# Attention outputs written channels by time in two 64-column halves of the PE array, their last rows placed by small DMAs

## What is computed

```python
# q, k, v, alpha: (4 batches, 8 heads, 768 steps, 48 channels)
for t in range(S):
    state = alpha[:, :, t, :, None] * state + einsum('bhd,bhe->bhde', k[:, :, t], v[:, :, t])
    y[:, :, t] = einsum('bhd,bhde->bhe', q[:, :, t], state)
x = y.transpose(0, 2, 1, 3).reshape(3072, 384)
x = (((x @ w1) * (x @ w2)) @ w3) @ w_out              # 384 -> 1024 -> 1024 -> 384
for e in range(4):                                    # p: the tokens' shares of the experts
    out += p[:, e:e + 1] * (np.maximum(x @ w1[e], 0) @ w2[e])
```

## Time and profile before

| | |
|---|---|
| median of 3 runs | 1300.9 us (1299.86, 1300.90, 1301.36) |
| span of the profiled execution | 1299.8 us |
| PE busy | 1274.5 us (98%), 6954 matmul instructions |
| PEld / DVE / ACT / POOL busy | 1170.7 / 525.1 / 310.5 / 290.5 us |
| granted TensorE clock, mean | 0.996 of full speed |
| attention outputs (L880, L884), PE busy in the records | 32.8 and 54.0 us |
| transposes of the outputs (L891) | 72 instructions, 12.3 us |

### The profile page before, as it was taken

How to read it: one execution, slowest core, us unless ns; L and a number is a source line. 1 busy time by engine, 2 the same in 40 slices (tenths; PEclk the granted TensorE clock), 3 DMA queues, 4 the chain that set the end, 5 groups by cost and what they waited for, 6 DMA issues and landing times.

```text
span 1299.8 us, 18234 instructions
## 1 busy us (share of the span) xinstructions
PE 1274.5 (98%) x6954; PEld 1170.7 (90%) x6954; DVE 525.1 (40%) x1160; ACT 310.5 (24%) x581; POOL 290.5 (22%) x236
## 2 busy tenths in 40 slices
PE   7989999999999998999999999999999999999999
PEld 4679999999999997999999999999999999999998
DVE  6786868777797311222222222222222222222222
ACT  2343333433343421111111111111111111111111
POOL 4455435444354623000000000000000000000000
PEclk9999999999999999999999999999999999999999
DMA  7432222323224231111111111111111111221101
GB/s 243 100 80 51 75 73 49 85 49 76 70 49 102 74 141 55 65 65 65 65 65 65 65 65 65 65 65 65 66 65 65 65 65 49 74 73 70 61 16 49
DMA packets 45725, 93.12 MB, mean 72 GB/s; under 512 B 3808, under 2 KB 14560, under 8 KB 45664
## 3 DMA queue, kind: packets, MB, share of 16 engines
q1 hardware_dynamic: 45664, 92.34, 23.8%
HBM read 78.17 MB, written 14.16 MB: 71 GB/s over the span
## 4 chain that ended last, share of the span: by engine, by line
PE 87%; DVE 7%; issue 2%; ACT 2%; POOL 1%; DMA 1%; DVEq 0%; SPq 0%; POOLq 0%
PE bank L845 27%; PE bank L844 27%; PE bank L846 27%; PE bank L884 2%; DVE inputs L618 1%; DVE decay L631 1%; DVE keys_t L642 1%; PE bank L880 1%; POOL inputs L390 1%; DMA inputs<-akq 1%; PE bank L865 1%; ACT h_hi L472 1%; DVE scores L648 1%; PE bank L891 1%; PE bank L949 1%
## 5 line engine op out<-in xcount | busy, mean ns | idle before, releaser
L810 DVE SCALAR_TENSOR_TENSOR h_lo<-bank,h_hi 128x512 fp32r<-128x512 f32 x192 | 132.7, 691 | 620.4 <-ACT h_hi L586 620.4
L586 ACT ACTIVATE h_hi<-bank 128x512 fp32r<-128x512 f32 x192 | 114.8, 598 | 667.9 <-PE bank L846 667.9
L845 PE MATMUL bank<-we_lo,h_hi 128*128 128x384 f32 x768 | 257.1, 335 | 0.0
L846 PE MATMUL bank<-we_hi,h_lo 128*128 128x384 f32 x768 | 256.9, 335 | 0.0
L844 PE MATMUL bank<-we_hi,h_hi 128*128 128x384 f32 x768 | 256.3, 334 | 0.0
L844 PE MATMUL bank<-x_hi,we_hi 128*128 128x512 f32 x576 | 227.0, 394 | 3.2 <-issue 3.2
L845 PE MATMUL bank<-x_lo,we_hi 128*128 128x512 f32 x576 | 228.8, 397 | 0.0
L846 PE MATMUL bank<-x_hi,we_lo 128*128 128x512 f32 x576 | 228.1, 396 | 0.0
L384 POOL TENSOR_TENSOR we_lo<-staged,we_hi 128x512 f32 (+1 forms) x48 | 61.4, 1305 | 533.2 <-ACT we_hi L457 533.0
L844 PEld LDWEIGHTS bank<-we_hi,h_hi 128*128 128x128 f32 x768 | 144.3, 188 | 9.1
L845 PEld LDWEIGHTS bank<-we_lo,h_hi 128*128 128x128 f32 x768 | 144.2, 188 | 8.2
(11 more groups left out here) (85 smaller groups left out, 1483.9 us busy)
## 6 DMA issues: line engine op xcount, KB each, us to landing
x_hi<-x_hi_spill SPq DMA_DIRECT2D x24, 768.0 KB, 4.9
x_lo<-x_lo_spill SPq DMA_DIRECT2D x24, 768.0 KB, 6.5
staged<-wset SPq DMA_DIRECT2D x60, 256.0 KB, 6.4
inputs<-akq SPq DMA_DIRECT2D x48, 288.0 KB, 4.5
values<-v_rows SPq DMA_DIRECT2D x24, 192.0 KB, 4.9
x_hi_spill<-x_hi_out SPq DMA_DIRECT2D x8, 576.0 KB, 3.4
x_lo_spill<-x_lo_out SPq DMA_DIRECT2D x8, 576.0 KB, 4.8
w_sb<-w_t SPq DMA_DIRECT2D x16, 256.0 KB, 9.2
```

The source lines that it names most:

```text
L586: act.activation(h_hi[:, s % 2, :], bank[s % 2][:, :], ACT.Relu).then_inc(h_hi_ready, 1)
L810: dve.scalar_tensor_tensor(out=h_lo[:, s % 2, :], in0=bank[s % 2][:, :], scalar=0.0, in1=h_hi[:, s % 2, :], op0=ALU.max, op1=ALU.subtract) ...
L845: pe.matmul(dst, left[0], right[1], start=False, stop=False)
L846: return pe.matmul(dst, left[1], right[0], start=False, stop=last)
```

## The change

The products of `outputs` swap their sides: the weights are now 64 columns of `decayed` or `values` and the moving side is 128 columns of queries or scores, so that the result comes out channels by time. The even head of a pair goes to partitions 0 to 63 of bank 7 and the odd head to 64 to 127. A head has 48 channels and a half 64 places: host code pads the values with zeros to 64 (the load of a chunk's values grows from 192 to 256 KB), and a pair's four groups of 128 columns fill the bank. `y_copy`, `turn_outputs` and `y_sb`'s place are gone. ACT and DVE write pairs 0 to 2 directly into `x0`, and pair 3 into a buffer `rest`, from which six DMAs a chunk (each 16 partitions, high and low part, 16 KB) carry it to the unused partitions 48 to 63 and 112 to 127 of the three pairs; the rows of w1 and w2 are permuted on the host to match. `up1` of a tile now waits for these DMAs (`x0_moved`). The branch for gates out of range, which does not run on this data, is adapted too. The diff, cut to its core:

```diff
+REST = ODD - D
+MOVED = 16 * 6
+VD = HEADS * ODD
 ...
-        values = sb("values", [P, 2, DM], F32, first)
+        values = sb("values", [P, 2, VD], F32, first)
         keys_t = sb("keys_t", [P, PAIRS, P], F32, first)
-        y_sb = sb("y_sb", [P, DM], F32, first)
         state = sb("state", [PD, PAIRS, 2 * D], F32, first)
-        decayed = sb("decayed", [PD, PAIRS, 2 * D], F32, first)
+        decayed = sb("decayed", [PD, PAIRS, 2 * ODD], F32, first)
 ...
+        rest = sb("rest", [P, 2, CHUNK], F32R, first)
+        rest_hi, rest_lo = rest[:, 0], rest[:, 1]
 ...
+        x0 = [sb(f"x0_{t}", [P, 2, KT, TILE1], F32R, first) for t in range(TILES1)]
+        x0_hi, x0_lo = [x[:, 0] for x in x0], [x[:, 1] for x in x0]
 ...
+            def move_rest(b, c):
+                sp.wait_ge(x0_lo_ready, CHUNKS * b + c + 1)
+                t, i = divmod(c, CHUNKS1)
+                at = slice(i * CHUNK, (i + 1) * CHUNK)
+                for k in range(KT):
+                    for row in range(2):
+                        sp.dma_start(x0[t][row * ODD + D:(row + 1) * ODD, :, k, at].bitcast(F32),
+                                     rest[row * ODD + k * REST:row * ODD + (k + 1) * REST, :, :].bitcast(F32)).then_inc(x0_moved, 16)
 ...
             load_chunk(0, 2)
+            move_rest(0, 0)
             load_pieces(0, 1)
 ...
                 load_chunk(into_b, into_c)
+                move_rest(b, c)
 ...
             load_after(BATCH - 1, 3, BATCH - 1, 5)
-            for q in range(PIECES // 2):
+            load_pieces(1, 0)
+            move_rest(BATCH - 1, 4)
+            load_pieces(1, 1)
+            load_pieces(1, 2)
+            move_rest(BATCH - 1, 5)
+            for q in range(3, PIECES // 2):
                 load_pieces(1, q)
 
-            sp.wait_ge(x0_lo_ready, BATCH * CHUNKS)
+            sp.wait_ge(x0_moved, MOVED * BATCH * CHUNKS)
 ...
-            def y_copy(b, c):
+            def x0_high(b, c):
                 act.wait_ge(y_done, CHUNKS * b + c + 1)
-                act.activation(y_sb[:, :], bank[7][:, 0:DM], ACT.Copy).then_inc(y_ready, 1)
-
-            def x0_high(b, c):
-                act.wait_ge(y_turned, CHUNKS * b + c + 1)
                 t, i = divmod(c, CHUNKS1)
-                act.activation(x0_hi[t][:, :, i * CHUNK:(i + 1) * CHUNK],
-                               bank[7][:, 0:DM].rearrange("p (k t) -> p k t", k=KT), ACT.Copy).then_inc(x0_hi_ready, 1)
+                y = bank[7][:, :].rearrange("p (a t) -> p a t", a=PAIRS)
+                act.activation(x0_hi[t][:, :, i * CHUNK:(i + 1) * CHUNK], y[:, 0:KT], ACT.Copy)
+                if not (isinstance(b, int) and b == 0 and c == 0):
+                    act.wait_ge(x0_moved, MOVED * (CHUNKS * b + c))
+                act.activation(rest_hi, y[:, KT], ACT.Copy).then_inc(x0_hi_ready, 1)
 ...
                     if chunk and s % 2:
-                        y_copy(*chunk)
                         x0_high(*chunk)
 ...
+                    dve.tensor_tensor(new_state, new, decayed[:, :, :].rearrange("p a (r e) -> p a r e", r=2)[:, :, :, 0:D],
+                                      ALU.add).then_inc(state_summed, 1)
 ...
-                    dve.tensor_tensor(decayed[rows, :, cols], state[rows, :, cols],
+                    dve.tensor_tensor(decayed[rows, :, row * ODD:row * ODD + D], state[rows, :, cols],
 ...
-                dve.tensor_tensor(x0_lo[t][:, :, at], bank[7][:, 0:DM].rearrange("p (k t) -> p k t", k=KT), x0_hi[t][:, :, at],
-                                  ALU.subtract).then_inc(x0_lo_ready, 1)
+                y = bank[7][:, :].rearrange("p (a t) -> p a t", a=PAIRS)
+                dve.tensor_tensor(x0_lo[t][:, :, at], y[:, 0:KT], x0_hi[t][:, :, at], ALU.subtract)
+                dve.tensor_tensor(rest_lo, y[:, KT], rest_hi, ALU.subtract).then_inc(x0_lo_ready, 1)
 ...
+                    heads = values[:, c % 2, pair * 2 * ODD:(pair + 1) * 2 * ODD].rearrange("p (r e) -> p r e", r=2)[:, :, 0:D]
+                    mm = pe.matmul(bank[7][0:PD, pair * 2 * D:(pair + 1) * 2 * D].rearrange("p (r e) -> p r e", r=2),
+                                   keys_t[:, pair, 0:PD], heads, start=True, stop=True)
 ...
+                    tiles = [bank[7][row * ODD:(row + 1) * ODD, pair * CHUNK:(pair + 1) * CHUNK] for row in range(2)]
                     if c >= 1:
-                        pe.matmul(bank[7][:, pair * 2 * D:(pair + 1) * 2 * D], inputs[:, c % 2, Q, pair, :], decayed[:, pair, :],
-                                  start=True, stop=False)
+                        for row in range(2):
+                            pe.matmul(tiles[row], decayed[:, pair, row * ODD:(row + 1) * ODD], inputs[:, c % 2, Q, pair, :],
+                                      start=True, stop=False)
                     for row in range(2):
-                        at = slice((2 * pair + row) * D, (2 * pair + row + 1) * D)
-                        mm = pe.matmul(bank[7][:, at], scores[:, pair // 2, pair % 2 * 2 + row, :], values[:, c % 2, at],
-                                       start=(c == 0), stop=(c == 0 or row == 1))
+                        at = slice((2 * pair + row) * ODD, (2 * pair + row + 1) * ODD)
+                        mm = pe.matmul(tiles[row], values[:, c % 2, at], scores[:, pair // 2, pair % 2 * 2 + row, :], start=(c == 0), stop=True)
                 mm.then_inc(y_done, 1)
-
-            def turn_outputs(b, c):
-                pe.wait_ge(y_ready, CHUNKS * b + c + 1)
-                for k in range(KT):
-                    mm = pe.transpose(bank[7][:, k * P:(k + 1) * P], y_sb[:, k * P:(k + 1) * P], identity[:, :])
-                mm.then_inc(y_turned, 1)
 
             def up1(b, s, which, wait_x0):
                 t, f = divmod(s % STEPS1, FT)
                 if which == 0:
                     if f == 0 and wait_x0:
-                        pe.wait_ge(x0_lo_ready, CHUNKS * b + CHUNKS1 * (s // FT + 1))
+                        pe.wait_ge(x0_moved, MOVED * (CHUNKS * b + CHUNKS1 * (s // FT + 1)))
 ...
-            steps = (score, state_products, outputs, turn_outputs)
-            first_beside = {4: (0, 1), 5: (2,), 6: (3,)}
-            second_beside = {3: (1, 0, 1), 6: (1, 2), 8: (1, 3), 18: (2, 0, 1), 22: (2, 2), 25: (2, 3)}
+            steps = (score, state_products, outputs)
+            first_beside = {4: (0, 1), 5: (2,)}
+            second_beside = {3: (1, 0, 1), 6: (1, 2), 18: (2, 0, 1), 22: (2, 2)}
 ...
+    v_rows = np.pad(v_rows, ((0, 0), (0, 0), (0, 0), (0, REST))).reshape(BATCH * CHUNKS, P, VD)
+    x0_rows = [(2 * k + row) * D + i if i < D else (2 * KT + row) * D + k * REST + i - D
+               for k in range(KT) for row in range(2) for i in range(ODD)]
 ...
-        "wset0": weight_set(moe_w1, moe_w2),
+        "wset0": weight_set(moe_w1[x0_rows], moe_w2[x0_rows]),
```

More of the change, by code:

```diff
@@ L40 @@
 KT, FT = DM // P, FF // P
+assert REST * KT == D and KT == PAIRS - 1
 ALPHA_LOW, ALPHA_HIGH = 0.75, 1.0
@@ L117, in gated_attention_experts @@
         wp_lo = sb("wp_lo", [P, FT, DM], F32R, first)
-        x0_hi = [sb(f"x0_hi{t}", [P, KT, TILE1], F32R, first) for t in range(TILES1)]
-        x0_lo = [sb(f"x0_lo{t}", [P, KT, TILE1], F32R, first) for t in range(TILES1)]
+        x0 = [sb(f"x0_{t}", [P, 2, KT, TILE1], F32R, first) for t in range(TILES1)]
+        x0_hi, x0_lo = [x[:, 0] for x in x0], [x[:, 1] for x in x0]
         a_sb = sb("a_sb", [P, 2, TILE1], F32, first)
@@ L149, in gated_attention_experts @@
         redo_product = scores[0:PD, :, :, :].rearrange("p i a t -> p (i a t)")[:, 0:SEQ]
+        y_sb = keys_t[:, :, :].rearrange("p a t -> p (a t)")[:, 0:DM]
         redo_y = values[:, :, :].rearrange("p i d -> p (i d)")[:, 0:CHUNKS * 2 * D].rearrange("p (c e) -> p c e", c=CHUNKS)
@@ L182, in gated_attention_experts @@
         y_done = sem("y_done")
-        y_ready = sem("y_ready")
-        y_turned = sem("y_turned")
         x0_hi_ready = sem("x0_hi_ready")
         x0_lo_ready = sem("x0_lo_ready")
+        x0_moved = sem("x0_moved")
         a_done = sem("a_done")
@@ L528, in _ @@
             split_high(0, 1)
-            y_copy(0, 0)
             x0_high(0, 0)
@@ L535, in _ @@
             check(0, 2)
-            y_copy(0, 1)
             fold_high(4)
@@ L543, in _ @@
             check(0, 3)
-            y_copy(0, 2)
             pieces_high(0, 4)
@@ L577, in _ @@
                             act.wait_ge(redo_turned, CHUNKS * b + c)
-                        act.dma_start(y_sb[:, :], redo_dram[:, c].rearrange("p a e -> p (a e)")).then_inc(redo_y_loaded, 16)
+                        y_rows = y_sb.rearrange("p (k r e) -> p k r e", k=KT, r=2)
+                        act.dma_start(y_rows[:, :, :, 0:D].rearrange("p k r e -> p (k r) e"),
+                                      redo_dram[:, c, 0:KT].rearrange("p a (r e) -> p (a r) e", r=2)).then_inc(redo_y_loaded, 16)
+                        for row in range(2):
```

(20 more changed lines are left out.)

8 lines of the change are left out of this document (5 added, 3 removed).

## The result

The changed kernel takes **1338.3 us** (median of 4 runs, 1337.4 to 1339.2) against 1301.1 (4 runs, 1299.9 to 1302.3): ratio 1.028, 95% interval 1.027 to 1.030. It is 37 us slower. The forecast was 8 us slower, 1309, with a range to 1325; the sign was right and the size was not.

The account below looks back on a forecast made before the run. PE, busy 98% of the span, was taken as the bound, with DVE second beside the attention. Second tiles +0.9, first tiles +3.4 and the start +3.8 summed to +8.1 us, giving 1309.0 us, range 1294 to 1325.

Parts of the forecast that it names:

- The transposes and the waits for `y_sb`: Work removed on PE: 7.9 us of transposes and 5.8 us of waits, 13.7 us at the most.
- The halves overlap: Output products on PE: both array halves work at once, block 1.94 us, saving 0.66 us a chunk.
- rival B: Output products' halves run one after the other: block 3.5 us, total 1318 us; chance 0.12.
- The second subtraction on DVE: In each `x0_low` on DVE, the added subtraction was taken to cost 0.2 us.
- the signs: What would show the forecast right, among them DVE without idle before `g_product` beside chunks 0 to 2.
- Rival A: Moves take no more than PE's own road, so no wait at tiles: -13 us, 1288; chance 0.17.
- The start: First tile: chunk 2's `x0_low` ends at 72.45, moved at 76.3 against 73.20; 3.1 + 3.5 clock - 2.8 waits, +3.8 us.
- The lag, 3.85 us: From `x0_lo` to `x0_moved`: five issues of 0.35 us on SP plus a 2.1 landing, ends 2.8 and 5.0.
- rival C: Clock falls at the seven later tile boundaries too, 3.5 us each: three falls 1319, all 1333; chance 0.15.
- The step that what is queued behind that wait waits "for later events anyway": SP's queue behind the wait for `x0_lo_ready`: tile stores or next chunk's loads wait for later events anyway; no cost counted.
- Second tiles: Boundary of each batch's second tile, four of them: 1.4 us sooner, lag +1.63, net +0.2 each, +0.9 in all.
- First tiles: First tile of the next batch, three of them: 0.25 us sooner, lag +1.38, net +1.1 each, +3.4 in all.

Follow-up runs that it names:

- e1_no_moves: Changed kernel without the six small DMAs a chunk, SP only passing the semaphore on, output incomplete: 1291.0 us, ratio 0.993 to the kernel before.
- e7_early_x0: Changed kernel with e3_piece_order's load order, and ACT and DVE writing `x0` and `rest` earlier in each chunk: 1293.5 us, ratio 0.9955 to the kernel before.
- e4_fill_wait: Changed kernel with unread matmuls on PE before each wait for `x0_moved`, 18 in the loop and 36 at the start: 1327.6 us.
- e3_piece_order: Changed kernel with SP issuing the last batch's weight-piece loads ahead of the moves of chunks 3, 4 and 5: 1325.1 us.
- e6_half_moves: Changed kernel with only the even heads' three of six moves per chunk, output incomplete: 1306.9 us, ratio 1.005 to the kernel before.
- e9_one_half_at_a_time: e7_early_x0 with all output products of one head of the pairs ahead of the other's, instead of alternating: 1312.4 us.

## Why the prediction went wrong

*Right.* The sign, and its mechanism: PE's savings are real and are spent on waiting for the moves. The transposes and the waits for `y_sb` went. The halves overlap: 1.77 us and the edges, 1.91 in all, where 1.94 was forecast, so rival B is out. The second subtraction on DVE costs 0.2 us (`rest` ends at 128.31, `x` at 127.55 + 0.56 = 128.11). DVE's two idle times beside chunks 0 to 2 (0.32 and 0.53 us) are gone, as the signs said. Rival A's working, without the lag, gave 1288; e1_no_moves measured 1291.0 and e7_early_x0 1293.5.

*The start, right by luck.* PE's first matmul of tile 1 came 3.6 us late, where 3.1 was forecast for it (3.8 with the clock and the waits that absorb part), and the first of its next `up1` 3.4 late (82.49 against 79.12). But `rest` ended at 71.26 and not at 72.45, and the lag there was 5.5 us and not 3.85: two errors that cancel. What the clock alone cost there, for which 3.5 was forecast, isn't shown: with the clock kept up (e4_fill_wait) tile 1 starts 1.8 us later and is 3.5 shorter.

*The lag, 3.85 us.* It was built as five issues of 0.35 and a landing of 2.1. The landing was near enough (1.8), the issue was not: 0.63. The measured lag is 5.2, above even the upper end of 5.0. The nearest row was a load of another kind, and that the issue "could be nearly free" was a guess in the wrong direction. At eight boundaries this is 8 x 1.35 = 11 us.

*The clock, rival C.* The forecast had the clock fall at the start alone, with rival C at 0.15. It fell at five of the six boundaries in the loop with a wait of 3.5 us, and in the last batch. The forecast's wait of 2.45 us lay between a row without a fall and a row with one; the real one, 3.5 us with the longer lag, no longer lay between. Rival C's price for one fall, 3.5 us, was too high for the loop: it was taken from a stretch of light work, and e4_fill_wait shows 1.6 to 1.9 each, 8.3 in all. C with its price at all seven would have given 1333 and came nearest, but partly by luck: the price was twice the real one and stood in for the lag and for SP's queue.

*SP's queue in the last batch.* The step that what is queued behind that wait waits "for later events anyway" holds in the loop and fails behind it, where the queue holds weight pieces that wait for nothing that is late. The prediction looked at `load_pieces` at the start and not at the end. It cost 13 us by e3_piece_order: lag, clock and pieces of that boundary, and the stretch behind it.

*The sum, mended.* Second tiles: forecast +0.2, and 1.35 for the lag and 1.6 for the clock make 3.2; measured 2.6 (with the clock's fall of the start in it), 3.6 and 4.1 for the first three. First tiles: 1.1 + 1.35 + 1.6 = 4.1; measured 4.1, 4.2, 4.2. Over the run: 8.1 as forecast, 10.8 for the lag, 8.3 for the clock, and 7.9 for the last batch (8.6 less the 0.2 and 1.35, and the 0.8 behind it) make 35.1 of the measured 35.8. So the working of PE's savings against DVE's pace stands within about 1 us a tile; two terms and one place were missing.

*And where the moves stood.* The prediction took the end of `x0_low` as given and asked how long the DMAs are. In the kernel before 2.2 to 2.5 us lay behind it, and nothing asked for more. The outputs stood in their bank at about 122 us, though, and `x0_low` ended at 128.3 behind 16 transposes of 5.3 us that, as e7_early_x0 shows, can wait. With the order changed on ACT and DVE the issues and landings cost nothing at the boundaries of the loop; the start keeps its wait of 6.4 us.

## What to carry to other kernels

A transfer that is put between two engines needs its lead time moved ahead with it: look not only at the slack before the consumer, but at how long the data have been ready before the producer got to them, and put the producer's step there. Count small DMAs one by one on the queue that issues them, at the price of their own kind, and read that queue's program to its end. A wait that lowers the clock costs more than it seems: here most waits of 3.5 us were followed by slow work that cost another 1.6 to 1.9, and waits of 1.5 us before the same tiles were not, so the first microseconds taken off such a wait are worth the most.

## What was not expected of the hardware

- Issuing a 16 KB transfer from SBUF to SBUF takes SP 0.63 us; a load of 192 KB takes 0.35, and one of 256 KB in the changed kernel as well. One run per partition instead of two changes it to 0.61, half the partitions to 0.73. It lands 1.8 us after its issue (median of 144; 2.7 in e7_early_x0). By the Trainium skill, "DMA: Bandwidth & Descriptors", on the anatomy of a DMA issued by GpSimd, a transfer has some 2.0 us fixed, most of it at the receipt of the write, and the sequencer's dispatch is about 0.05 of it. These are issued by SP: the landing is near the page's figure, the issue is twelve times its dispatch.
- Idle PE and the clock, in rows of this case: after waits of 1.5 us (e6_half_moves) and 1.0 us (e3_piece_order) the granted clock stayed at 1.00; after 3.51 us PE's records show the 1.2 GHz level from 133.49 to 136.85. The length of one wait doesn't decide it alone: after 3.45 us at 421.82, and after 3.50 us in e3_piece_order (307.39), the clock did not fall, and in e6_half_moves it fell after 2.48 us (442.23).
- Two halves of 64 columns run float32 products at once, with the same 128 or 112 rows in both. The Trainium skill, "TensorE: Matmul & The Clock Gate", part 3, ties the overlap of a weight load with a running matmul to different row groups; 32 loads and 32 streams in 1.77 us speak against that here.
- Where the order of the queue changes from one half to the other (e9_one_half_at_a_time, 122.70), four records of `decayed` start from 122.70 on, ahead of the four of `values` at 122.92: the first product of the second half starts beside the last `decayed` product of the first, although a `values` product stands between them in the program.
